# Attention with two gated MLPs on one core: three score products instead of four, one scaling copy less per query head, and another order of the first loads

## The chip, the cores and the metric

The kernel runs on one core of a Trainium2 chip. The metric is the device time of one execution in microseconds, lower is better. Before the change three executions took 1159.36, 1161.23 and 1161.65 us (median 1161.23).

## What is computed

Four batches of eight heads with 576 positions and head size 64, then two MLPs over the 2304 tokens. All arrays are float32.

```python
def _attn_ref(q, k, v, tau):
    scale = 1.0 / np.sqrt(q.shape[-1])
    scores = scale * np.matmul(q, k.transpose(0, 1, 3, 2))
    thresh = np.max(scores, axis=-1, keepdims=True) - tau
    scores = np.where(scores >= thresh, scores, -1000000000.0)
    scores = scores - np.max(scores, axis=-1, keepdims=True)
    attn = np.exp(scores)
    attn = attn / (np.sum(attn, axis=-1, keepdims=True) + 1e-09)
    return np.matmul(attn, v)
# x = attention as [tokens, 512]; x = gate1(x @ w_in) @ w_out; x = gate2(x @ w2_in) @ w2_out
# gate1(h) = h * clip(h + 3, 0, 6) / 6; gate2(h) = h * sigmoid(1.702 * h); hidden size 2048
```

## The kernel before, in words

**Precision.** TensorE multiplies fp32r values, which hold less than float32. Every operand is therefore split: a high part is the value rounded to fp32r, a low part is what the rounding left. A product of two split operands is then made of several matmuls that add up in one PSUM bank: high by high, high by low, low by high.

**The score product.** A head is only 64 rows deep and the array 128, so the kernel puts the query twice into the 128 partitions, and the key too (`load_q`, `load_k`: two transfers each, one per half of the partitions). For a query head three operations make `q_sp`: ScalarE's `high_q` (L700) writes the rounded, scaled query, negated in rows 0 to 63 (scale column `q_hi_scale`); ScalarE's `scale_q` (L704) multiplies `q_raw` by `q_in_scale`, which is 0 in rows 0 to 63 and the scale in rows 64 to 127; GpSimd's `low_q` (L851) subtracts the one from the other. What is left is the high part in rows 0 to 63 and the low part in rows 64 to 127. For a key head ScalarE's `high_k` (L709) and GpSimd's `low_k` (L856) write `k_hi` and `k_lo`, each with the same content in both halves. One matmul of `q_sp` with `k_hi` and one with `k_lo`, both over 128 rows, give all four products (L451).

**Slots.** The 32 heads are taken in 16 pairs. A pair has nine slots of 128 queries: four of its first head, a middle slot (MID) in which the last 64 queries of the first head and the first 64 of the second share the tile, and four of the second head. A slot has four score matmuls of 288 columns (two halves of the keys, `k_hi` and `k_lo`), the MID slot eight: 320 with `k_hi` and 320 with `k_lo` in all 144 slots. Each engine has its program written out by hand, slot by slot, and semaphores tie them. In iteration g of that loop, TensorE makes the scores of slot g+2, turns the masked exponentials of slot g-2 (five 128x128 transposes into `tr`, L466), multiplies a finished group of turned columns by the values (L480) and, from slot 46 on, adds one piece of the first MLP (twelve matmuls of 288 columns, L489 or L498). VectorE takes the row maximum (L590), the mask with its sum (L598) and the low part of the turned columns (L616). ScalarE takes the exponential (L720), the high part of the turned columns (L725) and the high parts of heads, values, weights and x. GpSimd makes the thresholds (L867) and the other low parts.

**Queues around the change.** There are two score buffers, so the scores of slot g+2 wait for the mask of slot g. SyncE issues all transfers; `load_q(h)` and `load_k(h)` wait until head h-2 has been split. Before slot 0 SyncE issues tau, q of head 0, k of head 0, waits for the constants, then v, k and q of head 1. ScalarE starts with L700, L704 and L709 of head 0, takes two exponentials, and then head 1. GpSimd makes the low parts of q and k of head 0, two thresholds, then head 1. TensorE begins when both low parts of head 0 are done. In the loop, pair i+1 is prepared in pair i: `high_k` in slots 2 and 6, `high_q` in 3 and 7, `scale_q` in 4 and 8. At the end of a pair VectorE inverts the nine sums (L605, L607), and TensorE turns them with a transpose whose weight load has nine columns (L459).

**After the attention** (from about 500 us) the rest of the two MLPs runs as plain tiles; no instruction of the change lies there.

The two constants that the split of a query needs:

```python
for half, scale in ((0, -float(HD) ** -0.5), (HD, float(HD) ** -0.5)):
    rows = slice(half, half + HD)
    dve.tensor_scalar(q_hi_scale[rows, :], tau_raw[rows, :], 0.0, scale, ALU.is_ge, ALU.mult)
    dve.tensor_scalar(q_in_scale[rows, :], tau_raw[rows, :], 0.0, max(scale, 0.0), ALU.is_ge, ALU.mult)
```

Of the kernel before, what the change touches and what calls it, by code (L numbers as in the profile page):

```python
# [7 lines left out]
ALU = mybir.AluOpType  # L8
# [3 lines left out]
P = 128  # L12
# [8 lines left out]
def attention_moe_kernel(nc, qT, kT, v, tau, w1_in, w1_out, w2_in, w2_out, out):  # L21
# [81 lines left out]
    with ExitStack() as ctx:  # L103
# [7 lines left out]
        three = sb("three", [P, 1])  # L111
        stage = sb("stage", [P, 2, UNIT])
# [18 lines left out]
        q_hi_scale = sb("q_hi_scale", [P, 1], where=att)  # L131
        q_in_scale = sb("q_in_scale", [P, 1], where=att)
# [38 lines left out]
        q_scaled = sem("q_scaled")  # L171
# [100 lines left out]
        def _(sp):  # L272
            def load_q(h):
                wait(sp, q_lo_done, h - 1)
                for half in range(2):
                    sp.dma_start(q_raw[half * HD:half * HD + HD, h % 2, :], qT[h]).then_inc(q_loaded[h % 2], 16)

            def load_k(h):
                wait(sp, k_lo_done, h - 1)
                for half in range(2):  # L280
                    sp.dma_start(k_raw[half * HD:half * HD + HD, h % 2, :], kT[h]).then_inc(k_loaded[h % 2], 16)
# [153 lines left out]
        def _(pe):  # L435
            def scores(g):
                i, s = divmod(g, SLOTS)
                wait(pe, mask_done, g - 1)
                if s in (0, MID):
                    pe.wait_ge(q_lo_done, 2 * i + 1 + s // MID)  # L440
                    pe.wait_ge(k_lo_done, 2 * i + 1 + s // MID)
# [127 lines left out]
        def _(dve):  # L569
            dve.memset(q_sp[:, S:S + TAIL].bitcast(F32), 0.0).then_inc(consts_done, 1)  # L570
            dve.memset(prob[:, :, S:WIDE], 0.0).then_inc(consts_done, 1)
            dve.memset(v_raw[:, FULL, :], 0.0).then_inc(consts_done, 1)
            dve.memset(three[:, :], 3.0).then_inc(consts_done, 1)
# [4 lines left out]
            for half, scale in ((0, -float(HD) ** -0.5), (HD, float(HD) ** -0.5)):  # L578
                rows = slice(half, half + HD)
                dve.tensor_scalar(q_hi_scale[rows, :], tau_raw[rows, :], 0.0, scale, ALU.is_ge, ALU.mult  # L580
                                  ).then_inc(tau_done, 1)
                dve.tensor_scalar(q_in_scale[rows, :], tau_raw[rows, :], 0.0, max(scale, 0.0), ALU.is_ge, ALU.mult
                                  ).then_inc(tau_done, 1)
            dve.wait_ge(tau_done, 1)
            dve.tensor_tensor(tau_abs[:, :], tau_raw[:, :], tau_neg[:, :], ALU.max).then_inc(tau_done, 1)

# [100 lines left out]
        def _(act):  # L687
# [9 lines left out]
            def high_q(h):  # L697
                act.wait_ge(q_loaded[h % 2], 32 * (h // 2 + 1))
                heads_free(h)
                act.activation(q_place(h), q_raw[:, h % 2, :], ACT.Copy, scale=q_hi_scale[:, :]).then_inc(q_hi_done, 1)  # L700

            def scale_q(h):
                act.wait_ge(q_hi_done, h + 1)
# [266 lines left out]
```

## Time and profile before

| | |
|---|---|
| median of three executions | 1161.23 us (1159.36 to 1161.65) |
| the profiled execution | 1159.2 us, its span 1157.4 us |
| TensorE matmul busy | 1093.3 us, 94% |
| VectorE, ScalarE, GpSimd busy | 560.6, 550.1, 490.9 us |
| chain that ended last | TensorE 82%, VectorE 6%, issue 4%, ScalarE 4%, GpSimd 2%, DMA 1% |

The span runs from the first to the last instruction of the profiled execution. Busy time is the union of an engine's instructions; it does not say whether the engine was the one that others waited for. The chain goes back from the last instruction, at each step to what released it, and so tells which engine set the time in each stretch. In a row of the timeline the first number is the start in the span, the second the duration, and brackets hold the idle time of the engine before it and what ended it. TensorE's matmuls are pipelined: a duration is longer than the distance to the next start, and the distance is what a matmul costs in a dense stretch.

### The profile page before, as it was taken

To read this page: it belongs to the slowest core of one execution; us is meant where nothing else is said; L and a number is where in the kernel's file an instruction comes from. 1 tells how busy PE (TensorE), PEld (TensorE's weight loads), DVE (VectorE), ACT (ScalarE), POOL (GpSimd) and SP (SyncE) were. 2 spreads that over 40 slices of the span, in tenths; PEclk is the share of its full clock that TensorE was granted. 3 is DMA by queue.
4 is the path that set the end of the run, shared out by engine and by line. 5 is a ranking of instruction groups with operands and counts; after the bars stand their busy time and mean duration, and the time that the engine had idled before them with its cause. 6 is when DMAs were issued, how large, how long until landed. Compare 5 with 4: busy or idle time off the path is not lost.

```text
span 1157.4 us, 17664 instructions
## 1 busy us (share of the span) xinstructions
PE 1093.3 (94%) x6720; PEld 1027.0 (89%) x6720; DVE 560.6 (48%) x1038; ACT 550.1 (48%) x1034; POOL 490.9 (42%) x582
## 2 busy tenths in 40 slices
PE   4888799999999999878999999999999999999998
PEld 3767599999999989878999999999999999999997
DVE  3889788778877887224322222232222223222221
ACT  4788686867676776235423333333233223332221
POOL 3466655455645563268333332243333222222222
PEclk9999899999999999989999999999999999999999
DMA  3445563256335522454333211222221002222210
GB/s 109 120 129 151 137 143 103 77 134 169 89 93 134 144 74 77 114 139 141 112 119 118 88 60 54 83 91 91 92 91 55 28 28 82 83 82 82 82 55 27
DMA packets 90627, 112.36 MB, mean 97 GB/s; under 512 B 25120, under 2 KB 69296, under 8 KB 90544
## 3 DMA queue, kind: packets, MB, share of 16 engines
q1 hardware_dynamic: 90544, 111.25, 33.3%
q8 instruction: 53, 0.87, 0.3%
q14 instruction: 30, 0.25, 0.1%
HBM read 78.12 MB, written 33.10 MB: 96 GB/s over the span
## 4 chain that ended last, share of the span: by engine, by line
PE 82%; DVE 6%; issue 4%; ACT 4%; POOL 2%; DMA 1%; SPq 0%; ACTq 0%; POOLq 0%; DVEq 0%
PE mm L489 19%; PE score L500 17%; PE tr L489 13%; PE score L498 10%; PE score L451 7%; PE tr L466 6%; PE mm L480 5%; PE mm L498 5%; DVE prob L598 2%; DVE neg_max L590 2%; DVE pt_lo L616 1%; POOL w_lo L884 1%; ACT gate L749 1%; POOL g_lo L894 1%; DMA inv_b<-inv_scratch 1%
## 5 line engine op out<-in xcount | busy, mean ns | idle before, releaser
L894 POOL TENSOR_TENSOR g_lo<-act_f,g_hi 128x384 fp32r<-128x384 f32 (+1 forms) x208 | 197.7, 955 | 421.5 <-ACT g_hi L757 421.5
L489 PE MATMUL mm<-x_hi,w_hi 128*128 128x384 f32 (+1 forms) x512 | 163.7, 320 | 7.9 <-DVE x_lo L622 7.9
L489 PE MATMUL mm<-x_hi,w_lo 128*128 128x384 f32 (+1 forms) x512 | 162.8, 318 | 0.0
L489 PE MATMUL mm<-x_lo,w_hi 128*128 128x384 f32 (+1 forms) x512 | 162.7, 318 | 0.0
L725 ACT ACTIVATE pt_hi<-tr 128x640 fp32r<-128x640 f32 x144 | 101.7, 706 | 96.5 <-PE tr L466 95.7
L752 ACT ACTIVATE gate<-mm 128x384 f32<-128x384 f32 x48 | 23.6, 492 | 220.5 <-PE mm L489 220.5
L451 PE MATMUL score<-k_hi,q_sp 128*128 128x288 f32 x320 | 98.8, 324 | 29.9 <-DVE prob L598 18.6
L616 DVE TENSOR_TENSOR pt_lo<-tr,pt_hi 128x640 fp32r<-128x640 f32 x144 | 118.3, 821 | 16.2 <-ACT pt_hi L725 14.9
L590 DVE TENSOR_REDUCE neg_max<-score 128x1 f32<-128x576 f32 x144 | 108.2, 751 | 31.1 <-PE score L451 28.3
L867 POOL TENSOR_SCALAR thresh<-neg_max,tau_abs 128x1 f32<-128x1 f32 x144 | 42.0, 292 | 186.3 <-DVE neg_max L590 185.4
L466 PE MATMUL tr<-ident,prob 128*128 128x128 f32 x720 | 106.9, 281 | 14.7 <-issue 12.3
L598 DVE SCALAR_TENSOR_TENSOR prob<-score,thresh,prob 128x576 f32<-128x576 f32 x144 | 116.3, 808 | 0.0
L720 ACT ACTIVATE prob<-score,neg_max 128x576 f32<-128x576 f32 x144 | 106.4, 739 | 13.7 <-DVE neg_max L590 12.9
L500 PE MATMUL score<-w_lo,g_hi 128*128 128x512 f32 x288 | 112.3, 390 | 0.0
L500 PE MATMUL score<-w_hi,g_lo 128*128 128x512 f32 x288 | 112.2, 390 | 0.0
L500 PE MATMUL score<-w_hi,g_hi 128*128 128x512 f32 x288 | 112.0, 389 | 0.0
L757 ACT ACTIVATE g_hi<-act_f 128x384 fp32r<-128x384 f32 (+1 forms) x208 | 102.6, 493 | 8.7 <-DVE act_f L630 6.2
L466 PEld LDWEIGHTS tr<-ident,prob 128*128 128x128 f32 x720 | 84.1, 144 | 24.8 <-issue 23.5
L489 PEld LDWEIGHTS mm<-x_hi,w_hi 128*128 128x128 f32 x512 | 96.7, 189 | 10.0 <-issue 8.1
L489 PE MATMUL tr<-x_hi,w_hi 128*128 128x384 f32 (+1 forms) x320 | 105.6, 330 | 0.0
L489 PE MATMUL tr<-x_lo,w_hi 128*128 128x384 f32 (+1 forms) x320 | 105.6, 330 | 0.0
L489 PE MATMUL tr<-x_hi,w_lo 128*128 128x384 f32 (+1 forms) x320 | 105.6, 330 | 0.0
(73 smaller groups left out, 2439.8 us busy)
## 6 DMA issues: line engine op xcount, KB each, us to landing
x_raw<-x_t_scratch SPq DMA_DIRECT2D x18, 768.0 KB, 6.2
q_raw<-in_qT SPq DMA_DIRECT2D x64, 144.0 KB, 2.9
k_raw<-in_kT SPq DMA_DIRECT2D x64, 144.0 KB, 2.8
stage<-in_w_in SPq DMA_DIRECT2D x16, 512.0 KB, 6.8
stage<-in_w_out SPq DMA_DIRECT2D x16, 512.0 KB, 7.1
o_parts_scratch<-o_t SPq DMA_DIRECT2D x32, 160.0 KB, 1.8
x_raw<-o_parts_scratch SPq DMA_DIRECT2D x16, 288.0 KB, 5.3
part<-o_parts_scratch SPq DMA_DIRECT2D x16, 288.0 KB, 6.2
```

Of the source, the lines that this page charges most:

```text
L451: m = pe.matmul(score[:, g % 2, half, 0:HALF], q_sp[:, col:col + P], k_part[:, side, half * HALF:half * HALF + HALF], start=e == 0, stop=e ...
L466: m = pe.transpose(turned_p[:, c * P:c * P + P], prob[:, x % PROBS, c * P:c * P + P], ident[:, :])
L489: m = pe.matmul(bank[:, 0:width], w[:, col:col + P], x[:, k, 0:width], start=(k == 0 and e == 0), stop=(k == KC - 1 and e == 2))
L498: r = pe.matmul(bank[:, 0:width], w[:, col + m * P:col + m * P + P], g[:, c, 0:width], **ends)
L500: r = pe.matmul(bank[:, :], g[:, c, m * P:m * P + P], w[:, col:col + DM], **ends)
L590: dve.tensor_reduce(neg_max[:, r:r + 1], score[:, g % 2, :, 0:HALF], AX.XY, ALU.max, negate=True).then_inc(max_done, 1)
L598: dve.scalar_tensor_tensor(out=p, in0=score[:, g % 2, :, 0:HALF], scalar=thresh[:, r:r + 1], in1=p, op0=ALU.is_ge, op1=ALU.mult, accum_out ...
L616: dve.tensor_tensor(pt_place(pt_lo, x), turned_place(x), pt_place(pt_hi, x), ALU.subtract).then_inc(pt_lo_done, 1)
L720: act.activation(prob[:, g % PROBS, 0:S].rearrange("p (a n) -> p a n", a=2), score[:, g % 2, :, 0:HALF], ACT.Exp, bias=neg_max[:, r:r + 1] ...
L725: act.activation(pt_place(pt_hi, x), turned_place(x), ACT.Copy).then_inc(pt_hi_done, 1)
L757: act.activation(g_hi[:, c, 0:width], act_f[:, c % 2, 0:width], ACT.Copy).then_inc(g_hi_done, 1)
L894: pool.tensor_tensor(g_lo[:, c, 0:width], act_f[:, c % 2, 0:width], g_hi[:, c, 0:width], ALU.subtract).then_inc(g_lo_done, 1)
```

## The change

- The scale 1/8 goes into the high parts of both sides. `q_scale` is 1 in rows 0 to 63 and the scale in rows 64 to 127, `k_scale` the other way round. `high_q` writes the rounded value with that column, and `low_q` subtracts only rows 0 to 63. `q_sp` then holds the low part, not scaled, above, and the scaled high part below; `k_hi` holds the scaled high part above and the plain one below. `scale_q` is gone.
- `k_lo` is valid only in rows 64 to 127, and the matmul with it takes these 64 rows alone. Low by low is no longer computed: three products instead of four. The number of matmuls and their columns stay as they were.
- `high_k` has a scale column now. The first key head is split by VectorE.
- q and k of a head come by one transfer each, whose source gives each row twice. The first loads stand in the order q0, tau, k0, k1, q1.
- ScalarE makes one exponential of a constant column before anything else. On ScalarE and GpSimd, head 1 stands ahead of the first exponentials and thresholds.

```diff
-                for half in range(2):
-                    sp.dma_start(q_raw[half * HD:half * HD + HD, h % 2, :], qT[h]).then_inc(q_loaded[h % 2], 16)
+                sp.dma_start(q_raw[:, h % 2, :], both_halves(qT[h])).then_inc(q_loaded[h % 2], 16)
...
+            load_q(0)
             sp.dma_start(tau_raw[:, :], tau.broadcast_to([P, 1])).then_inc(tau_loaded, 16)
-            load_q(0)
             load_k(0)
+            load_k(1)
+            load_q(1)
             sp.wait_ge(consts_done, 8)
             load_v(0)
-            load_k(1)
-            load_q(1)
...
-                parts = [(side, col, k_part) for side, col in sides for k_part in (k_hi, k_lo)]
+                parts = [(side, col, k_part, rows) for side, col in sides for k_part, rows in ((k_hi, 0), (k_lo, HD))]
                 for half in range(2):
-                    for e, (side, col, k_part) in enumerate(parts):
-                        m = pe.matmul(score[:, g % 2, half, 0:HALF], q_sp[:, col:col + P],
-                                      k_part[:, side, half * HALF:half * HALF + HALF],
+                    for e, (side, col, k_part, rows) in enumerate(parts):
+                        m = pe.matmul(score[:, g % 2, half, 0:HALF], q_sp[rows:P, col:col + P],
+                                      k_part[rows:P, side, half * HALF:half * HALF + HALF],
...
+            dve.wait_ge(k_loaded[0], 16)
+            dve.tensor_scalar(k_hi[:, 0, :], k_raw[:, 0, :], k_scale[:, :], None, ALU.mult).then_inc(first_k_hi_done, 1)
+            dve.wait_ge(first_k_hi_done, 1)
+            dve.tensor_tensor(k_lo[:, 0, :], k_raw[:, 0, :], k_hi[:, 0, :], ALU.subtract).then_inc(first_k_lo_done, 1)
...
-            def scale_q(h):
-                act.wait_ge(q_hi_done, h + 1)
-                act.activation(q_raw[:, h % 2, :], q_raw[:, h % 2, :], ACT.Copy, scale=q_in_scale[:, :]).then_inc(q_scaled, 1)
...
-                act.activation(k_hi[:, h % 2, :], k_raw[:, h % 2, :], ACT.Copy).then_inc(k_hi_done, 1)
+                act.activation(k_hi[:, h % 2, :], k_raw[:, h % 2, :], ACT.Copy, scale=k_scale[:, :]).then_inc(k_hi_done, 1)
...
+            act.activation(warm[:, :], three[:, :], ACT.Exp)
             act.wait_ge(tau_done, 6)
             high_q(0)
-            scale_q(0)
-            high_k(0)
+            high_k(1)
+            high_q(1)
             exponent(0)
             exponent(1)
-            high_k(1)
-            high_q(1)
-            scale_q(1)
...
-                pool.wait_ge(q_scaled, h + 1)
-                pool.tensor_tensor(q_sp[:, first:first + S], q_raw[:, h % 2, :], q_sp[:, first:first + S], ALU.subtract
-                                   ).then_inc(q_lo_done, 1)
+                pool.wait_ge(q_hi_done, h + 1)
+                pool.tensor_tensor(q_sp[0:HD, first:first + S], q_raw[0:HD, h % 2, :], q_sp[0:HD, first:first + S],
+                                   ALU.subtract).then_inc(q_lo_done, 1)
...
             low_q(0)
-            low_k(0)
+            low_k(1)
             threshold(0)
             threshold(1)
-            low_k(1)
             low_q(1)
```

The start of ScalarE's program, with the semaphores that each instruction waits for, before and then with the change:

```order
L700 ACT_TABLE_LOAD [waits q_loaded0,tau_done]
L700 ACTIVATE q_sp<-q_raw,q_hi_scale 128x576 [waits consts_done]
L704 ACTIVATE q_raw<-q_raw,q_in_scale 128x576 [waits q_hi_done]
L709 ACTIVATE k_hi<-k_raw 128x576 [waits k_loaded0]
L720 ACTIVATE prob<-score,neg_max 128x576 [waits max_done] x2
L709 ACTIVATE k_hi<-k_raw 128x576 [waits k_loaded1]
L700 ACTIVATE q_sp<-q_raw,q_hi_scale 128x576 [waits q_loaded1]
L704 ACTIVATE q_raw<-q_raw,q_in_scale 128x576 [waits q_hi_done]
L720 ACTIVATE prob<-score,neg_max 128x576 [waits max_done] x2
```

```order
L774 ACT_TABLE_LOAD
L774 ACTIVATE warm<-three 128x1 [waits consts_done]
L717 ACTIVATE q_sp<-q_raw,q_scale 128x576 [waits q_loaded0,tau_done]
L722 ACTIVATE k_hi<-k_raw,k_scale 128x576 [waits k_loaded1]
L717 ACTIVATE q_sp<-q_raw,q_scale 128x576 [waits q_loaded1]
L733 ACTIVATE prob<-score,neg_max 128x576 [waits max_done] x4
```

The table load has left the place behind the first query's arrival and waits for nothing; the key of head 0 is gone from ScalarE, and head 1 stands ahead of the first exponentials.

GpSimd behind its constants, before and then with the change (L851 and L859 are `low_q`, L856 and L864 `low_k`, L867 and L875 the threshold):

```order
L851 TENSOR_TENSOR q_sp<-q_raw,q_sp 128x576
L856 TENSOR_TENSOR k_lo<-k_raw,k_hi 128x576
L867 TENSOR_SCALAR thresh<-neg_max,tau_abs 128x1 x2
L856 TENSOR_TENSOR k_lo<-k_raw,k_hi 128x576
L851 TENSOR_TENSOR q_sp<-q_raw,q_sp 128x576
```

```order
L859 TENSOR_TENSOR q_sp<-q_raw,q_sp 64x576
L864 TENSOR_TENSOR k_lo<-k_raw,k_hi 128x576
L875 TENSOR_SCALAR thresh<-neg_max,tau_abs 128x1 x2
L859 TENSOR_TENSOR q_sp<-q_raw,q_sp 64x576
```

The first key split (k of head 0) left for VectorE; the one that stands second now is head 1's, and it stands ahead of the first threshold.

ScalarE in slots 7 and 8 of the first pair, where the second head of the next pair is prepared, before and then with the change:

```order
L700 ACTIVATE q_sp<-q_raw,q_hi_scale 128x576
L725 ACTIVATE pt_hi<-tr 128x5x128
L720 ACTIVATE prob<-score,neg_max 128x576
L704 ACTIVATE q_raw<-q_raw,q_in_scale 128x576
L731 ACTIVATE o_t<-mm 128x320
L725 ACTIVATE pt_hi<-tr 128x5x128
```

```order
L717 ACTIVATE q_sp<-q_raw,q_scale 128x576
L738 ACTIVATE pt_hi<-tr 128x5x128
L733 ACTIVATE prob<-score,neg_max 128x576
L744 ACTIVATE o_t<-mm 128x320
L738 ACTIVATE pt_hi<-tr 128x5x128
```

The scaling copy between the exponential and `o_t` is gone, and nothing else moved.

## Rows read from the trace of the kernel before

**Rows 1.** Windows: per stretch its us, busy per engine (x instructions), PEclk, DMA, GB/s

```profile
10.00:33.00 23.00, 16.57 (x64) 14.17 (x65) 13.26 (x24) 11.34 (x18) 7.86 (x13) 1.00 0.33 93
60.00:90.00 30.00, 26.01 (x168) 21.28 (x168) 27.35 (x53) 25.58 (x43) 19.58 (x26) 1.00 0.49 136
145.00:205.00 60.00, 59.05 (x451) 57.36 (x450) 49.04 (x97) 44.30 (x82) 32.84 (x47) 1.00 0.47 124
```

**Rows 2.** Timeline of the start: start us, us, engine line op, names, shapes [idle before <-releaser]

```profile
0.74 0.40 SPq L357 DMA_DIRECT2D tau_raw<-in_tau  x1
1.20 1.18 SPq L276 DMA_DIRECT2D q_raw<-in_qT  x2
...
4.05 0.16 DVE L585 TENSOR_TENSOR tau_abs<-tau_raw,tau_neg 128x1 f32<-128x1 f32 x1
...
4.80 1.28 ACT L700 ACT_TABLE_LOAD   x1 [4.80 <-DMA q_raw<-in_qT]
...
6.09 0.77 ACT L700 ACTIVATE q_sp<-q_raw,q_hi_scale 128x576 fp32r<-128x576 f32 x1
...
7.85 1.40 POOL L851 TENSOR_TENSOR q_sp<-q_raw,q_sp 128x576 fp32r<-128x576 f32 x1 [5.95 <-ACT q_raw L704]
9.21 1.40 POOL L856 TENSOR_TENSOR k_lo<-k_raw,k_hi 128x576 fp32r<-128x576 f32 x1
...
10.75 0.58 PE L451 MATMUL score<-k_hi,q_sp 128*128 128x288 f32 x1 [10.75 <-POOL k_lo L856]
...
11.37 0.44 PE L451 MATMUL score<-k_hi,q_sp 128*128 128x288 f32 x1
...
11.61 0.44 PE L451 MATMUL score<-k_lo,q_sp 128*128 128x288 f32 x1
```

**Rows 3.** Transfers into q_raw up to 40 us, and the window from 3 to 4 us

```profile
DMA to landing us min/median/max: 2.7/2.9/3.0
...
3.00:4.00 1.00, 0.00 (x0) 0.00 (x0) 0.46 (x5) 0.00 (x0) 0.00 (x0) 1.00 0.78 251
```

**Rows 4.** Timeline, the same VectorE operation alone and beside a GpSimd operation

```profile
199.49 0.17 DVE L605 TENSOR_SCALAR total_e<-total 128x9 f32<-128x9 f32 x1
...
229.66 0.65 DVE L605 TENSOR_SCALAR total_e<-total 128x9 f32<-128x9 f32 x1
...
229.47 0.81 POOL L894 TENSOR_TENSOR g_lo<-act_f,g_hi 128x288 fp32r<-128x288 f32 x1 [0.79 <-ACT g_hi L757]
```

**Rows 5.** Groups by line and shape: busy us, mean ns of one | idle before

```profile
L622 DVE TENSOR_TENSOR x_lo<-x_raw,x_hi 128x384 fp32r<-128x384 f32 x72 | 51.2, 769 | 18.0 <-ACT x_hi L744 18.0
...
L704 ACT ACTIVATE q_raw<-q_raw,q_in_scale 128x576 f32<-128x576 f32 x32 | 24.7, 772 | 0.1
L700 ACT ACTIVATE q_sp<-q_raw,q_hi_scale 128x576 fp32r<-128x576 f32 x32 | 24.6, 770 | 0.0
L709 ACT ACTIVATE k_hi<-k_raw 128x576 fp32r<-128x576 f32 x32 | 21.9, 684 | 0.0
```

**Rows 6.** Waits from 145 to 470 us: us in total, times, longest

```profile
PE score L451 <- DVE prob L598: 8.0, 11, 1.2
```

**Rows 7.** Timeline of ScalarE, VectorE and TensorE around one of these waits

```profile
426.72 0.78 ACT L704 ACTIVATE q_raw<-q_raw,q_in_scale 128x576 f32<-128x576 f32 x1
...
427.86 0.49 DVE L622 TENSOR_TENSOR x_lo<-x_raw,x_hi 128x288 fp32r<-128x288 f32 x1 [0.41 <-ACT x_hi L744]
...
430.17 0.40 PE L451 MATMUL score<-k_hi,q_sp 128*128 128x288 f32 x1 [0.86 <-DVE prob L598]
```

**Rows 8.** Timeline of TensorE, dense, around the transpose with nine weight columns

```profile
443.67 0.29 PE L451 MATMUL score<-k_hi,q_sp 128*128 128x288 f32 x1
443.80 0.29 PE L451 MATMUL score<-k_lo,q_sp 128*128 128x288 f32 x1
443.93 0.27 PE L459 MATMUL tr<-ident,inv_total 128*9 128x128 f32 x1
444.04 0.71 PE L466 MATMUL tr<-ident,prob 128*128 128x128 f32 x5
```

More of the change, by code:

```diff
@@ L130, in attention_moe_kernel @@
         tau_abs = sb("tau_abs", [P, 1], where=att)
-        q_hi_scale = sb("q_hi_scale", [P, 1], where=att)
-        q_in_scale = sb("q_in_scale", [P, 1], where=att)
+        q_scale = sb("q_scale", [P, 1], where=att)
+        k_scale = sb("k_scale", [P, 1], where=att)
         q_raw = sb("q_raw", [P, 2, S], where=att)
@@ L272, in _, with both_halves @@
         def _(sp):
+            def both_halves(rows):
+                return bass.AP(tensor=rows.tensor, offset=rows.offset, ap=[[0, 2]] + [list(a) for a in rows.ap])
             def load_q(h):
                 wait(sp, q_lo_done, h - 1)
-                for half in range(2):
-                    sp.dma_start(q_raw[half * HD:half * HD + HD, h % 2, :], qT[h]).then_inc(q_loaded[h % 2], 16)
+                sp.dma_start(q_raw[:, h % 2, :], both_halves(qT[h])).then_inc(q_loaded[h % 2], 16)
             def load_k(h):
-                wait(sp, k_lo_done, h - 1)
-                for half in range(2):
-                    sp.dma_start(k_raw[half * HD:half * HD + HD, h % 2, :], kT[h]).then_inc(k_loaded[h % 2], 16)
+                if h == 2:
+                    sp.wait_ge(first_k_lo_done, 1)
+                else:
+                    wait(sp, k_lo_done, h - 2)
+                sp.dma_start(k_raw[:, h % 2, :], both_halves(kT[h])).then_inc(k_loaded[h % 2], 16)
             def load_v(h):
@@ L440, in scores @@
                     pe.wait_ge(q_lo_done, 2 * i + 1 + s // MID)
-                    pe.wait_ge(k_lo_done, 2 * i + 1 + s // MID)
+                    if g == 0:
+                        pe.wait_ge(first_k_lo_done, 1)
+                    else:
+                        pe.wait_ge(k_lo_done, 2 * i + s // MID)
                 if s < MID:
@@ L572, in _ @@
             dve.memset(v_raw[:, FULL, :], 0.0).then_inc(consts_done, 1)
-            dve.memset(three[:, :], 3.0).then_inc(consts_done, 1)
             dve.wait_ge(tau_loaded, 16)
-            dve.tensor_scalar(tau_neg[:, :], tau_raw[:, :], -1.0, None, ALU.mult).then_inc(tau_done, 1)
[L578 to L584, printed above, removed]
+            for tile, half in ((q_scale, HD), (k_scale, 0)):
+                rows, others = slice(half, half + HD), slice(HD - half, P - half)
+                dve.tensor_scalar(tile[rows, :], tau_raw[rows, :], 0.0, float(HD) ** -0.5, ALU.is_ge, ALU.mult
+                                  ).then_inc(tau_done, 1)
+                dve.memset(tile[others, :], 1.0).then_inc(tau_done, 1)
+            dve.tensor_scalar(tau_neg[:, :], tau_raw[:, :], -1.0, None, ALU.mult).then_inc(tau_done, 1)
+            dve.wait_ge(tau_done, 5)
             dve.tensor_tensor(tau_abs[:, :], tau_raw[:, :], tau_neg[:, :], ALU.max).then_inc(tau_done, 1)
+            dve.wait_ge(k_loaded[0], 16)
+            dve.tensor_scalar(k_hi[:, 0, :], k_raw[:, 0, :], k_scale[:, :], None, ALU.mult).then_inc(first_k_hi_done, 1)
+            dve.wait_ge(first_k_hi_done, 1)
+            dve.tensor_tensor(k_lo[:, 0, :], k_raw[:, 0, :], k_hi[:, 0, :], ALU.subtract).then_inc(first_k_lo_done, 1)
             def row_max(g):
@@ L791, in _ @@
                         high_q(2 * i + 2)
-                    if s == 4 and i + 1 < PAIRS:
-                        scale_q(2 * i + 2)
                     if s == 5:
@@ L799, in _ @@
                         high_q(2 * i + 3)
-                    if s == 8 and i + 1 < PAIRS:
-                        scale_q(2 * i + 3)
                     if s in (0, 5) and 0 < i <= UNITS:
```

13 lines of the change are left out of this document (8 added, 5 removed).

## The prediction
> **What bounds the kernel now.** I read the windows first, for how full each engine is in each stretch, then the timeline of the start, then the waits and the timeline of the stretch in which attention and MLP are mixed. Three stretches matter. Before the first matmul everything is a serial chain, and TensorE starts at 10.75 us [rows 2]. From there to about 145 us (46 slots, no MLP work) VectorE is the fullest engine, 27.35 of 30 us, with TensorE at 26.01 and ScalarE at 25.58 [rows 1]. From 145 to about 470 us (98 slots) TensorE is busy 59.05 of 60 us, ScalarE only 44.30 [rows 1]. Behind that no instruction of the change runs. So ScalarE, from which the change takes most, bounds no long stretch; what counts is the start, the few waits of TensorE, and whether the score matmuls still cost what they did.
>
> **Part 1: the start.** Before: tau goes first (issued 0.74), q0 second (1.20); the table load sits behind q0's landing at 4.80 and takes 1.28, then L700 (0.77), `scale_q` and `high_k` on ScalarE, then 1.40 + 1.40 us of GpSimd, then TensorE at 10.75 [rows 2]. After, each step at its duration in these rows:
> - q0 is issued at 0.74 in one transfer. A transfer of 144 KB took 2.9 us from its issue; one of 288 KB needs at the 251 GB/s of the loading phase some 0.6 us more [rows 3]. q0 lands at about 4.2, tau right behind it, 4.3. k0 is limited by the same rate: 1.2 us later, 5.4. k1 follows at 6.6, q1 at 7.8.
> - The table load waits for nothing and is over long before 4.3: 1.28 us go off the path. The exponential of one column hides there too.
> - Six small VectorE operations took until 4.21 from tau's landing, some 0.7 us (the last ran from 4.05 for 0.16) [rows 2]. ScalarE's L700 then runs from 5.0 to 5.8, and GpSimd's `low_q` from 5.9 for 1.40 us. It has half the rows, but the same columns, so I take the same duration: 7.3. `scale_q`, 0.77, is gone from the path.
> - VectorE splits k0 beside that: two operations of 576 columns. The nearest row is 769 ns for a subtraction of 384 columns, in a mean that includes waiting [rows 5]; I take 0.7 us each, from 5.45 to 6.9.
> - The second of them and `low_q` want SBUF at the same time. The addition to nine sums takes 0.17 us alone and 0.65 us when a GpSimd subtraction started 0.19 us before it, and it ends as that one ends [rows 4]. So one of the two waits for the other: the later one ends at about 8.0 in place of 7.3. The Trainium skill (SBUF — State Buffer, "SBUF: two separate sides") says that a VectorE operation with two SBUF inputs and a GpSimd operation take the shared port pair as an exclusive lock; by it alone the start would be at about 8.1, without it at 7.4. The row agrees.
> - First matmul at 7.9, against 10.75: **-2.9 us**. Ends: 7.4 if the two do not meet and the transfers land as early as small ones did (-3.4), 8.8 if both meet in full and k0 lands 0.7 us later (-2.0).
>
> Behind the first matmul two things are queued that were not. ScalarE has k1 and q1 (0.77 each, k1's landing 6.6) ahead of the first exponential: done at 8.6, while the first row maximum cannot be there before 9.9. GpSimd has `low_k(1)` (1.40) ahead of the first threshold: from 8.0 to 9.4, again before 9.9. Cost nothing; if k1 lands over 0.5 us late the difference comes back as delay of slot 0.
>
> **Part 2: slots without MLP work.** 11 of the 32 `scale_q` lie here. VectorE at 91% is the bound and loses no instruction. I read a whole pair on the timeline: ScalarE had ended `scale_q` before the transposes that it waits for next were done, in slots 4 and 8 alike. 0 us.
>
> **Part 3: slots with MLP work.** TensorE waited 8.0 us here in 11 places, all ahead of scores whose mask was late [rows 6]. A wait gets shorter only if ScalarE was late because of `scale_q`. One case is in rows 7: `scale_q` at 426.72, then x's high part, VectorE idle 0.41 us for it, and the scores 0.86 us late: 0.41 us come back. Two more places on the timeline have such a VectorE idle, 0.15 and 0.22 us; in the others VectorE had no idle time before the late mask, since it was inverting the sums. **-0.8 us**. Bounds: 0, if the next wait ends as late; -5.4, if each wait with a `scale_q` in its slot gave back up to the 0.67 us between two starts on ScalarE.
>
> **Part 4: what is added or only moved.** `high_k` gets a scale column: 770 ns with one (L700), 684 without (L709) [rows 5], so 31 times 0.09 us on ScalarE, which has over 15 of 60 us free in the mixed stretch: 0. In all ScalarE loses 24.7 us and gains 2.7. The first key is split by VectorE, in idle time. One transfer in place of two moves the same bytes and saves SyncE about 0.6 us each (1.18 for two [rows 2]); no transfer of q or k is waited for behind the start: 0.
>
> **Part 5: the matmul with 64 rows.** 320 of the 640 score matmuls use rows 64 to 127 only. Their columns stay 288, and in a dense stretch the distance between two starts is 0.13 us for 288 columns [rows 8], so fewer rows gain nothing. They alternate with matmuls of 128 rows, which makes 640 changes of the array's shape. No row of this kernel shows a change of rows. The nearest is a change of columns: the transpose with nine weight columns starts 0.13 us behind the score matmul, as all do, and the next starts 0.11 us behind it [rows 8]. Nothing is lost there, and I take 0. The other end is below, as a rival. The Trainium skill (TensorEngine Tiling (Array Packing), "Key Properties") says that a change of the tiling mode drains TensorE, and it lists both kinds as modes. For columns the rows speak against it; for rows no row here shows it. By that rule the sum would be rival A's.
>
> **Sum.** -2.9 - 0.8 = -3.7 us: the profiled execution, 1159.2 us, becomes 1155.5. That execution is 2.0 us below the median of 1161.23; the four known times lie at 1159.2 and 1159.36 and at 1161.23 and 1161.65, two and two. I put the forecast for a median between: 1156.5 us (1155.5 by the one base, 1157.5 by the other). About 0.2%, 2.3 us, is what a measurement can tell from no change. Own range of this case: 1153 to 1159.
>
> **Rival A, slower: the change of rows stops TensorE.** Before each change the array would first have to give out what is in it. Price per change, from rows: a matmul takes 0.29 us to its results where the next starts after 0.13, so a full drain costs 0.16; a matmul behind an idle time took 0.40 in place of 0.29, so a restart costs 0.11 [rows 7, 8]. In the mixed slots TensorE is the bound; they hold 98 x 4 + 11 x 4 = 436 changes: 48 us at 0.11. All 640 at 0.16 make 102 us. The time would be 1156.5 + 48 = 1204 up to 1258, and for a shorter stop of p us about 436 to 640 p more. It decides from p = 3.7 / 640 = 0.006 us on. For it: two shapes alternate in one accumulation, which this kernel never did. Against: rows 8. Chance of a p over 0.006: 0.23, of which 0.09 below 0.04 us.
>
> **Rival B, slower: the clock.** At 11 us 288 columns took 0.24 us, the level of 1.2 GHz; later they take 0.13, the level of 2.4 GHz [rows 2, 8]; the mean matmul is busy for 0.26 us from 10 to 33 us (16.57 for 64) and for 0.15 from 60 to 90 (26.01 for 168) [rows 1]. On the timeline the change comes after 31 us, when the value products had begun. Half as many rows at work might put it off. Some 37 slots without MLP work lie behind it; each has 4.4 score matmuls that would be 0.11 slower, 0.5 us, and the row maximum waits for them: up to 18 us, about 1174. Against: TensorE is busy for the same share of the time. Chance 0.05.
>
> **Rival C, nothing to be seen.** The start is earlier but the gain is eaten: the clock rises at the same absolute time, so some 3 us more run at the low level (0.5 us), k0 and `low_q` meet in full (0.9 us less), and the mixed slots give nothing: -3.7 + 0.5 + 0.9 + 0.8 = -1.5, or 1159.7. Chance 0.14.
>
> **How the numbers follow.** Forecast 0.58, rivals A 0.23, B 0.05, C 0.14. Faster by over 0.2% (below 1158.9): 0.95 of the forecast's 0.58 and a sixth of C, 0.58. Slower (over 1163.5): A without its smallest stops, and B, 0.26. The rest, 0.16, within 0.2%. The range starts at 1153 and reaches to 1176, a stop of 0.03 to 0.04 us per change or B's price; what is left out is 0.03 below and about 0.15 above, the large stops of A.
>
> **What would show it.** Right: the first score matmul starts between 7.4 and 8.8; starts of score matmuls in a dense stretch remain 0.13 apart, with `k_hi` and with `k_lo`; ScalarE's busy time falls by some 22 us and TensorE's stays; the waits before scores in the mixed stretch drop by about 0.8 from 8.0 us. Wrong: distances over 0.14 at every change of rows (A), distances of 0.24 beyond 35 us (B), or a start before 8 with the 46th slot no earlier than before (C).

## The result, and the profile after

The changed kernel takes 1281.73 us (median of four, 1280.09 to 1284.99), the kernel before 1161.44 beside it: ratio 1.1039, 95% interval 1.1008 to 1.1069. It is 120 us slower, and outside the range given.

The page of the changed kernel, busy time by engine and the chain that ended last. In all views PE stands for TensorE's matmuls, PEld for its weight loads, DVE for VectorE, ACT for ScalarE, POOL for GpSimd and SPq for what SyncE issues; a window gives busy time in the order PE, PEld, DVE, ACT, POOL, then the granted clock (PEclk), the DMA share and GB/s.

```profile
span 1279.8 us, 17569 instructions
PE 1208.4 (94%) x6720; PEld 1059.7 (83%) x6720; DVE 570.2 (45%) x1040; ACT 529.3 (41%) x1002; POOL 488.0 (38%) x581
...
PE 85%; DMA 4%; DVE 4%; issue 3%; POOL 2%; ACT 1%; SPq 1%; ACTq 0%; DVEq 0%; POOLq 0%
```

ScalarE lost 21 us of busy time, as forecast. TensorE has as many matmuls as before and is busy 115 us longer. TensorE has 85% of the chain (82% before), and DMA rose from 1% to 4%. So two things are to be found: why TensorE takes longer for the same matmuls, and which transfers are waited for.

**TensorE.** The timeline of the changed kernel in a dense stretch answers to [rows 8]:

```profile
300.12 0.29 PE L500 MATMUL mm<-x_hi,w_lo 128*128 128x288 f32 x1
300.12 0.19 PEld L462 LDWEIGHTS score<-k_hi,q_sp 128*128 128x128 f32 x1
300.25 0.29 PE L462 MATMUL score<-k_hi,q_sp 128*128 128x288 f32 x1
...
300.47 0.18 PEld L462 LDWEIGHTS score<-k_lo,q_sp 64*128 64x128 f32 x1 [0.16 <-issue]
300.47 0.40 PE L462 MATMUL score<-k_lo,q_sp 64*128 64x288 f32 x1
300.80 0.19 PEld L462 LDWEIGHTS score<-k_hi,q_sp 128*128 128x128 f32 x1
300.80 0.40 PE L462 MATMUL score<-k_hi,q_sp 128*128 128x288 f32 x1
301.12 0.18 PEld L462 LDWEIGHTS score<-k_lo,q_sp 64*128 64x128 f32 x1
301.12 0.40 PE L462 MATMUL score<-k_lo,q_sp 64*128 64x288 f32 x1
301.45 0.14 PEld L477 LDWEIGHTS tr<-ident,prob 128*128 128x128 f32 x1
301.45 0.33 PE L477 MATMUL tr<-ident,prob 128*128 128x128 f32 x1
```

The starts are 0.22, 0.33, 0.32 and 0.33 us apart where they were 0.13 apart. Look at the weight loads. The load of the first score matmul (300.12) stands beside the matmul ahead of it, 0.13 us early. Every load behind a change of rows starts together with its own matmul and is no longer hidden. That the nine-column transpose costs nothing still holds: its successor starts 0.11 us behind it, at full rows on both sides.

```profile
304.40 0.28 PE L470 MATMUL tr<-ident,inv_total 128*9 128x128 f32 x1
304.51 0.60 PE L477 MATMUL tr<-ident,prob 128*128 128x128 f32 x4
```

**The transfers.** SyncE and the first matmul on the timeline of the changed kernel, which answers to [rows 2]:

```profile
0.73 0.71 SPq L281 DMA_DIRECT2D q_raw<-in_qT  x1
1.51 0.41 SPq L365 DMA_DIRECT2D tau_raw<-in_tau  x1
...
1.96 4.30 SPq L288 DMA_DIRECT2D k_raw<-in_kT  x2
...
6.30 5.43 SPq L281 DMA_DIRECT2D q_raw<-in_qT  x1
10.51 0.77 ACT L717 ACTIVATE q_sp<-q_raw,q_scale 128x576 fp32r<-128x576 f32 x1 [8.28 <-DVE tau_abs L596]
...
11.78 5.57 SPq L293 DMA_DIRECT2D v_raw<-in_v  x1
15.18 0.52 DVE L600 TENSOR_SCALAR k_hi<-k_raw,k_scale 128x576 fp32r<-128x576 f32 x1 [4.71 <-DMA k_raw<-in_kT]
...
16.64 0.58 PE L462 MATMUL score<-k_hi,q_sp 128*128 128x288 f32 x1 [16.64 <-DVE k_lo L602]
```

The first matmul starts at 16.64 us, not at 7.9. k0 landed at about 15.2 and q1 at 26.85, 20.55 us after its issue; the third slot (slot 2 of pair 0) began at 29.19 (14.60 before), since `high_q(1)` stands ahead of the first exponentials on ScalarE. The windows of the changed kernel show how little the 16 DMA engines did meanwhile, against the 251 GB/s of [rows 3]:

```profile
3.00:4.00 1.00, 0.00 (x0) 0.00 (x0) 0.00 (x0) 0.00 (x0) 0.00 (x0) 1.00 0.16 51
10.00:33.00 23.00, 6.56 (x13) 3.44 (x13) 5.48 (x12) 4.32 (x6) 5.01 (x6) 1.00 0.16 56
```

A share of 0.16 is two and a half of the 16 engines. What is queued behind such a transfer comes late too. Stores of attention's output, with their size and the median us from issue to landing (before: 1.8 us):

```profile
o_parts_scratch<-o_t SPq DMA_DIRECT2D x32, 160.0 KB, 8.0
```

**Where the 122 us lie.** From the start of the first score matmul of each pair on the timelines (pair 15 ends here with the start of its last slot); differences to the kernel before, in us, of one profiled execution each. Pairs 0 to 4 have no MLP work, 6 to 15 are mixed with it, and in pair 5 the mixing begins. The columns add up to the difference of the profiled spans. Executions of one kernel lie several us apart, so differences of 1 or 2 us in a span say nothing; a3's profiled execution, 1162.87 us, is among the slowest of its twelve. The kernels below the first row are those of the experiments.

| kernel | first matmul | pairs 0-4 | pair 5 | pairs 6-14 | pair 15 | behind | span |
|---|---|---|---|---|---|---|---|
| before, us | 10.8 | 116.3 | 36.4 | 269.6 | 27.0 | 697.3 | 1157.4 |
| changed | +5.9 | +40.6 | +10.0 | +59.1 | +5.9 | +1.0 | +122.4 |
| a1_rows128 | +5.9 | +35.7 | +8.8 | +37.0 | 0 | +1.4 | +88.8 |
| a2_two_loads | -2.0 | +40.4 | +0.4 | +54.1 | +5.9 | +1.5 | +100.3 |
| a3_both | -2.0 | +0.8 | +0.5 | +2.9 | 0 | +1.5 | +3.7 |
| b1_rows64 | 0 | +35.1 | +1.9 | +53.7 | +5.9 | -0.1 | +96.5 |
| b2_one_load | +7.5 | +37.4 | +7.6 | +41.2 | 0 | -0.1 | +93.6 |
| b3_spread | -0.1 | +0.6 | +0.3 | +0.2 | 0 | +0.8 | +1.7 |
| a4_grouped | -2.1 | +6.0 | +0.9 | +18.8 | +2.2 | +0.3 | +26.1 |
| c1_tau_first | -2.3 | -1.9 | +0.3 | +3.1 | 0 | +0.3 | -0.5 |

### The profile page after: what moved, and what is told of

Same layout as the page of the kernel before. It is cut to its first block, busy times and chain, and to the rows that moved or that the text cites. A ratio compares the mean times of both kernels' runs of the same rounds, so it can differ in the third digit from the quotient of the medians.

```text
span 1279.8 us, 17569 instructions
## 1 busy us (share of the span) xinstructions
PE 1208.4 (94%) x6720; PEld 1059.7 (83%) x6720; DVE 570.2 (45%) x1040; ACT 529.3 (41%) x1002; POOL 488.0 (38%) x581
## 4 chain that ended last, share of the span: by engine, by line
PE 85%; DMA 4%; DVE 4%; issue 3%; POOL 2%; ACT 1%; SPq 1%; ACTq 0%; DVEq 0%; POOLq 0%
PE mm L500 18%; PE score L511 15%; PE score L462 15%; PE tr L500 12%; PE score L509 10%; PE tr L477 5%; PE mm L509 5%; PE mm L491 5%; DVE prob L615 3%; DMA q_raw<-in_qT 2%; DMA o_parts_scratch<-o_t 1%; POOL w_lo L892 1%; POOL g_lo L902 1%; DMA inv_b<-inv_scratch 1%; DMA v_raw<-in_v 1%
## 5 line engine op out<-in xcount | busy, mean ns | idle before, releaser
L462 PE MATMUL score<-k_hi,q_sp 128*128 128x288 f32 x320 | 123.8, 387 | 42.4 <-DVE prob L615 23.0
L875 POOL TENSOR_SCALAR thresh<-neg_max,tau_abs 128x1 f32<-128x1 f32 x144 | 42.0, 292 | 281.3 <-DVE neg_max L607 280.9
L462 PE MATMUL score<-k_lo,q_sp 64*128 64x288 f32 x320 | 132.0, 413 | 0.0
L462 PEld LDWEIGHTS score<-k_hi,q_sp 128*128 128x128 f32 x320 | 63.0, 197 | 82.7 <-DVE prob L615 38.8
L477 PE MATMUL tr<-ident,prob 128*128 128x128 f32 x720 | 113.8, 291 | 9.3 <-issue 9.2
L615 DVE SCALAR_TENSOR_TENSOR prob<-score,thresh,prob 128x576 f32<-128x576 f32 x144 | 116.3, 807 | 6.5 <-ACT prob L733 6.5
```

The lines of the kernel that those rows point to most:

```text
L462: m = pe.matmul(score[:, g % 2, half, 0:HALF], q_sp[rows:P, col:col + P], k_part[rows:P, side, half * HALF:half * HALF + HALF], start=e == ...
L477: m = pe.transpose(turned_p[:, c * P:c * P + P], prob[:, x % PROBS, c * P:c * P + P], ident[:, :])
L615: dve.scalar_tensor_tensor(out=p, in0=score[:, g % 2, :, 0:HALF], scalar=thresh[:, r:r + 1], in1=p, op0=ALU.is_ge, op1=ALU.mult, accum_out ...
```

## Two causes, taken away one at a time

Theory 1: the change of rows costs some 0.2 us each. Theory 2: the single transfers, whose source repeats 64 rows, are served slowly.

**a1_rows128**: the changed kernel without the change of rows. The added rows multiply the unused half of `k_lo` with the low part of q, so the values differ; no work is left out.

```
-for k_part, rows in ((k_hi, 0), (k_lo, HD))
+for k_part, rows in ((k_hi, 0), (k_lo, 0))
```

> The changed kernel, but the matmul with k_lo takes all 128 rows again, so that all 640 score matmuls have one shape. (Rows 0 to 63 of k_lo hold no low part, so the values change; no work is left out.) Theory 1, each change between 64 and 128 rows costs TensorE about 0.19 us: score matmuls start 0.13 us apart in dense stretches, and some 105 us go (83 from 436 changes in mixed slots, the rest from the slots without MLP work): 1172 to 1182 us, still slower than before by the slow first loads. Rival, the slow transfers of q and k make the loss: above 1250 us.

**a2_two_loads**: the changed kernel with two transfers of 64 rows each for q and k.

```
-sp.dma_start(q_raw[:, h % 2, :], both_halves(qT[h]))
+for half in range(2):
+    sp.dma_start(q_raw[half * HD:half * HD + HD, h % 2, :], qT[h])
```

> The changed kernel, but q and k of a head come by two transfers of 64 rows each again; order of loads and all else as changed. Theory 2, a transfer whose source starts with a step of zero over two is served by few DMA engines: the first score matmul starts at 8 to 9 us in place of 16.6, slot 2 at 12 to 13 in place of 29.2, SyncE's issues take 0.6 us again, and the wait for v behind the first x loads shrinks; in all 18 to 27 us less than the changed kernel, 1255 to 1264 us. The distance between score matmuls stays 0.32. If the rival (transfers make the whole loss) holds: below 1175.

**a3_both**: both alterations together.

> Both: 128 rows for k_lo and two transfers of 64 rows. What is left of the change is the scale in the high parts, one ScalarE operation for a query, the first key on VectorE, the order of the first loads and the early table load. Both theories, and parts 1 to 3 of the prediction: 3.7 us under the kernel before, about 1157 to 1158 us, ratio 0.996 to 0.998, first score matmul at 7.4 to 8.8 us. If these parts are worth nothing: ratio 1.000.

Measured: a1 1248.04 us, a2 1259.51 (one run each), a3 1160.61, beside 1159.87 for the kernel before. a3's ratio is 0.9999 (0.9988 to 1.001): not the 3.7 us that parts 1 to 3 promised, but the other case, in which they are worth nothing. So the two causes together are the whole loss. Each alone costs 88 or 100 us, and both together 122, not 188. a2's time came as expected, though its slot 2 began at 14.71 us and not at 12 to 13. a1 fits neither expectation (it lies 2 us under the rival's): I had taken the loss of the transfers for a matter of the start. The waits of a1 from 12 to 470 us show a loss all along:

```profile
ACT v_hl L727 <- DMA v_raw<-in_v: 54.4, 12, 13.5
PEld tr L477 <- issue: 43.4, 32, 14.2
```

and its transfers, KB each and us to landing:

```profile
v_raw<-in_v SPq DMA_DIRECT2D x32, 16.0 KB, 9.2
```

ScalarE stands for v up to 13.5 us, and the evictions of the transposes stand behind it. In the changed kernel TensorE is slower, and the same late v is waited for less: 17.5 us in all, in 4 places. The causes overlap.

Part of what late transfers cost comes by way of TensorE's clock. Up to the last score matmul the granted clock was at half for 6.8 us in the kernel before, for 82 in a1, 96 in b2 (below) and 34 in the changed kernel; in a1 the first such stretches come behind idle times of TensorE of 2 to 3 us (from 51.3, 71.3 and 81.7 us), and the longest falls into one of 14.0 us (from 169.5). The same window in a1 and in the kernel before:

```profile
105.00:127.00 22.00, 18.07 (x97) 16.36 (x98) 16.08 (x31) 14.23 (x24) 11.64 (x16) 0.77 0.33 112
```

```profile
105.00:127.00 22.00, 18.92 (x123) 15.30 (x122) 20.56 (x39) 17.11 (x28) 13.38 (x17) 1.00 0.67 163
```

TensorE is almost as busy, with 97 matmuls in place of 123. It was busy for 54 us of a1's time at the low level, against 5 before; work at half the clock takes twice as long, so I estimate that up to 25 of the 88 us are of this kind (29 in b2, 10 in the changed kernel). No run takes the clock out by itself.

Put in the other way, each cause alone into the kernel before:

**b1_rows64**: the second score product over rows 0 to 63 only, which leaves out the product of the two low parts.

```
-m = pe.matmul(score[...], q_sp[:, col:col + P], k_part[:, side, ...]
+m = pe.matmul(score[...], q_sp[0:rows, col:col + P], k_part[0:rows, side, ...]
```

> The kernel before, with one edit: the matmul with k_lo takes rows 0 to 63 only (the high part of q; the product low by low is left out). The 64 rows lie at the other end of the array than in the change. Theory 1: score matmuls start 0.32 us apart in dense stretches, slot distance without MLP work about 2.95 in place of 2.54 us, 100 to 110 us slower than before, 1261 to 1272 us. If only the place in rows 64 to 127 costs: no change, 1161.

**b2_one_load**: the single transfers alone, in the kernel before.

> The kernel before with one alteration: q and k of each head come by one transfer whose source repeats 64 rows (its first dimension has two entries), in place of two. Theory (such a transfer is served by about two of the 16 DMA engines, at some 50 GB/s, holds SyncE for 3 to 6 us at its issue, and makes what is queued behind it late): 1230 to 1262, with q and k landing over 6 us after their issue and output stores landing at a median of over 6 us; first matmul later than 14 us. Rival (it costs only together with the changed order at the start, where four of them stand in a row): under 1180.

Measured: b1 1255.77 us, b2 1252.77 (one run each, the kernel before at 1159.87 and 1159.66). b1 is a little under its range; the timeline has the same distances as the changed kernel, with the other half of the array:

```profile
301.12 0.29 PE L451 MATMUL score<-k_hi,q_sp 128*128 128x288 f32 x1
301.35 0.39 PE L451 MATMUL score<-k_lo,q_sp 64*128 64x288 f32 x1
301.67 0.40 PE L451 MATMUL score<-k_hi,q_sp 128*128 128x288 f32 x1
302.00 0.39 PE L451 MATMUL score<-k_lo,q_sp 64*128 64x288 f32 x1
302.32 0.77 PE L466 MATMUL tr<-ident,prob 128*128 128x128 f32 x5
```

b2 lies within its range, so the rival (only together with the new order at the start) falls. Its start moved by 7.5 us although tau landed 2.6 us after its issue: q0 landed at 10.1 and k0 at 16.0, on the timeline:

```profile
10.13 1.28 ACT L701 ACT_TABLE_LOAD   x1 [10.13 <-DMA q_raw<-in_qT]
...
15.99 0.68 ACT L710 ACTIVATE k_hi<-k_raw 128x576 fp32r<-128x576 f32 x1 [2.98 <-DMA k_raw<-in_kT]
```

## What makes a matmul slow: the rows, or their change

**a4_grouped**: a2 with the score matmuls in another order, k_hi for both halves, then k_lo for both: as many 64-row matmuls, fewer changes.

```
-for half in range(2):
-    for e, (side, col, k_part, rows) in enumerate(parts):
+parts.sort(key=lambda x: x[3])
+for e, (side, col, k_part, rows) in enumerate(parts):
+    for half in range(2):
```

> The changed kernel with two 64-row transfers for q and k, and its score matmuls in another order: first the two halves with k_hi (128 rows), then the two with k_lo (rows 64 to 127). As many 64-row matmuls as before, but two changes of rows per slot in place of four. The same kernel with the halves alternating measured 1259.5, 98 us over the kernel before. Theory 1 (each change of rows costs about 0.2 us, since the weights of the next matmul are then not loaded ahead): half of it goes, 1204 to 1216; in a dense slot the starts stand 0.32, 0.13, 0.32, 0.13 us apart. Rival (each 64-row matmul is slow by itself, by twice that amount, and the changes are free): 1252 to 1264.

Measured: 1185.21 us (1184.77 to 1186.99), ratio 1.0226 (1.0208 to 1.0243). The rival (64-row matmuls are slow by themselves) falls; theory 1 stands, but its figure was at least 19 us too high. Three reasons. Slot 4 of a pair has eight score matmuls, and its changes fall from eight to two, so a pair has 18 changes in place of 40, not half. In pairs 0 to 4 the changes left, 18 of them at about 0.17 us, 3 us a pair, find room in TensorE's idle time, also some 3 us of a pair's 22.8: VectorE bounds them again, at 26.75 of 30 us, as before [rows 1]. And two changes in a row of like matmuls cost a dense slot 0.33 us and not 0.40, as the timeline below shows. Windows of a2 and of a4:

```profile
60.00:90.00 30.00, 27.29 (x137) 18.78 (x135) 22.84 (x44) 20.36 (x34) 16.22 (x21) 1.00 0.38 108
```

```profile
60.00:90.00 30.00, 27.25 (x160) 20.53 (x161) 26.75 (x51) 23.48 (x39) 19.68 (x25) 1.00 0.47 134
```

TensorE is equally busy in both, with 137 matmuls in a2 and 160 in a4: in a2 VectorE waits for it. a4's timeline, dense, where x2 joins two matmuls of the same shape:

```profile
300.37 0.42 PE L465 MATMUL score<-k_hi,q_sp 128*128 128x288 f32 x2
...
300.72 0.29 PEld L465 LDWEIGHTS score<-k_lo,q_sp 64*128 64x128 f32 x2 [0.16 <-issue]
300.72 0.53 PE L465 MATMUL score<-k_lo,q_sp 64*128 64x288 f32 x2
...
301.18 0.42 PEld L480 LDWEIGHTS tr<-ident,prob 128*128 128x128 f32 x4 [0.17 <-issue]
```

Two k_hi take 0.35 us to the next start, two k_lo 0.46. Over the mixed stretch the median distances are 0.13 from k_hi to k_hi, 0.22 to the first k_lo, 0.24 to the second, 0.22 to the transpose. I read this as two prices per change: 0.09 us in which the next matmul can't start, and 0.10 us of a weight load that stands in the open. The load of the second k_lo, where nothing changes, is hidden again: it starts at 300.83, its matmul at 300.96. A dense slot then has 0.33 us more than before (3.59 in place of 3.26), and the changed kernel 0.73 (3.99). Split in this way the two prices are an inference; that the sum belongs to the change is shown. a2 beside a4 settles it: from a k_lo to the transpose behind it takes 0.33 us in a2, where that k_lo itself follows a change, and 0.22 in a4, where it follows another k_lo; and in a2 the second k_hi, of 128 rows, is as slow to its successor (0.33) as any k_lo.

## What makes the transfer slow

**b3_spread**: the kernel before with single transfers of the same bytes and descriptors, whose source runs over the rows first and repeats second. Rows come to lie in pairs, so the values differ; no work is left out.

```
-ap=[[0, 2]] + [list(a) for a in rows.ap]
+ap=[list(rows.ap[0]), [0, 2], list(rows.ap[1])]
```

> The kernel before with q and k by one transfer each, of the same bytes and descriptors as in the other single transfer, but its source runs over the 64 rows first and repeats each row second (so partitions 2r and 2r+1 get row r, and the values computed are others; no work is left out). Theory (the first dimension of the pattern sets over how many DMA engines a transfer is spread: 2 entries give two engines, 64 give all): landings of 3 to 4 us as before, 1158 to 1163, ratio 0.997 to 1.002. Rival (a source that reads the same rows twice in one transfer is slow, or 128 descriptors in one transfer are): 1230 or more.

Measured: 1161.19 us, ratio 1.0014 (1.0004 to 1.0025). The rivals fall: 128 descriptors in one transfer and rows that are read twice cost at most 0.25% together, where b2 lost 8%. DMA up to 30 us, in b2 and in b3 (KB each, us to landing, and the queue's packets, MB and share of the 16 engines):

```profile
DMA packets 1324, 1.45 MB, mean 48 GB/s; under 512 B 761, under 2 KB 761, under 8 KB 1324
q1 hardware_dynamic: 1323, 1.45, 14.1%
```

```profile
DMA packets 2700, 3.28 MB, mean 109 GB/s; under 512 B 1504, under 2 KB 1504, under 8 KB 2700
q1 hardware_dynamic: 2700, 3.28, 40.0%
k_raw<-in_kT SPq DMA_DIRECT2D x5, 288.0 KB, 3.2
q_raw<-in_qT SPq DMA_DIRECT2D x4, 288.0 KB, 3.4
```

Each transfer of q or k took 3.2 to 3.4 us here, and its bytes came at up to 335 GB/s in a part of that window; with two entries in the first dimension the queue took 14% of the 16 engines, about two. The Trainium skill (DMA: Bandwidth & Descriptors, "Rules for kernel authors") says this too: an outermost dimension of c entries, a leading repetition among them, confines the whole transfer to at most c engines. The runs agree: from 4 to 6 us the DMA share was 0.13 in b2 and 0.98 in b3. SyncE is held as well: in the changed kernel its issues at the start took 3.7 to 5.6 us each once some transfers were queued, 0.6 us in b3.

## What is left of the gain, and where it goes

With both causes undone the start is 2.0 us earlier and nothing remains. I tried for a version that keeps it.

**c1_tau_first**: a3 with tau issued ahead of q0.

> The changed kernel with both costs undone (128 rows for k_lo, two transfers each for q and k), and tau issued first, ahead of q0. In the one with q0 first, tau was issued at 2.00 us, landed at about 4.8 and set the start of ScalarE (5.80) and the first matmul (8.79). Theory (the rest of the start is real but does not last): first matmul at 7.9 to 8.3, and yet 1158 to 1163, ratio 0.997 to 1.001, because the slots without MLP give the lead back. Rival (what is gained at the start stays): 2.4 to 2.8 us under the kernel before, ratio 0.9976 to 0.9979.

**d1_v_between**: the kernel before, with v's loads moved into the loads of x.

```
 for a in range(2):
+    if a == 1:
+        load_v(2 * i + 1)
     side = slice(a * HD, a * HD + HD)
```

> The kernel before with one move in SyncE's order: in each of the three places where six loads of x stand ahead of the two loads of v for the next head (288 KB each against 144 KB together), v goes between the third and the fourth of them. In the trace of before v landed 7.5 us after its issue there, ScalarE waited for it 4.8, 0.7 and 0.9 us, and at 133 us TensorE stood idle 5.56 us behind it. Theory (v's landing ends those waits, and the queue in front of it sets the landing): 1155 to 1158, 2 to 4.5 us below the kernel before; TensorE's idle time at 133 us falls to 1 to 4 us. Rival (x is wanted as early, and lands later by what v gains): within 1 us of the kernel before.

**d2_tau_v**: the same in c1.

> The same move of v's loads in the changed kernel with both costs undone and tau issued first. That one led the kernel before by 4.1 us at the fourth pair, and lost 2.2 us of it in the first slot of pair 9 (5.62 us in place of 3.47), where ScalarE waited 3.1 us for v and held up the transposes' evictions. Theory (late v loads take the lead away): slot 81 back to 3.4 to 4.0 us, the waits at 130 us shorter too, 1152 to 1156. Rival (the lead is lost wherever the next transfer or eviction is late): 1158 to 1161, level with the kernel before.

Measured: c1 1160.43 us, ratio 1.0011 (1.0 to 1.0022); d1 1162.24, ratio 1.001 (0.9999 to 1.0022); d2 1160.92, ratio 0.9999 (0.9988 to 1.001). c1 is level with the kernel before, as expected, but not for the reason given: the slots without MLP work kept its lead. The first matmul came at 8.47 us in c1, a little later than expected, since VectorE's first operation on k0 took 1.60 us beside GpSimd (0.52 in a3):

```profile
5.82 1.39 POOL L861 TENSOR_TENSOR q_sp<-q_raw,q_sp 64x576 fp32r<-64x576 f32 x1 [3.91 <-ACT q_sp L719]
5.93 1.60 DVE L602 TENSOR_SCALAR k_hi<-k_raw,k_scale 128x576 fp32r<-128x576 f32 x1 [1.47 <-DMA k_raw<-in_kT]
```

c1's lead grew from 2.3 to 4.1 us by the fourth pair, was 3.8 at pair 9, and 1.55 at pair 10. The growth was luck: in this execution TensorE reached the level of 0.13 us for 288 columns at 22.3 us, in d2, whose program is the same up to there, at 31.4, and d2's lead stayed at 2.3 over the first pair. A wait of c1 from 248.7 to 281.8 us:

```profile
ACT v_hl L729 <- DMA v_raw<-in_v: 3.1, 1, 3.1
```

In the kernel before the same wait was 0.7 us. A store of 160 KB had landed 3.5 us after its issue in place of 1.8, SyncE's loads of x wait for it, and v stands behind them. So 2.2 us of the lead are lost to a late transfer, and d2, with v earlier, loses only 0.4 there. But d1 and d2 show that v alone isn't the cause to remove: with v earlier, x is waited for. The waits of d1 from 118 to 260 us:

```profile
PE score L454 <- DVE prob L601: 7.2, 8, 3.8
DVE x_lo L625 <- ACT x_hi L747: 6.8, 7, 3.0
...
POOL x_raw L879 <- DMA inv_b<-inv_scratch: 4.9, 2, 4.6
```

TensorE's idle time of 5.56 us at 133 us became two, 1.62 us before 128.5 and 3.77 before 133.8, so hardly less in all, and the slot behind got longer (4.72 us in place of 3.51); the granted clock was at half for 10.2 us there, for 6.8 before. In d2 slot 81 took 3.87 us, within the expectation, and by then the lead was already down to 0.1. The rivals of d1 and d2 hold, d1 at 1.02 us from the kernel before. Part of d2's lead went between 60 and 90 us, where the granted clock was 0.92 (1.00 in c1); what puts a stretch of the lower level there I can't say. A lead of 2.3 us is thus as large as what such stretches add or take from one execution to the next.

## Why the prediction was wrong

- **Part 5, 0 us: the step that failed first.** I took a change of rows at nothing because a change of columns costs nothing. The changed kernel shows 0.20 us for a change inside the group and 0.09 for the first behind a dense stretch: 0.73 us in a dense slot, 100 us in a2. The rule of the Trainium skill (TensorEngine Tiling (Array Packing), "Key Properties"), that a change of the tiling mode drains TensorE, is borne out for rows by these timelines (0.09 us to the next start, and the weight load in the open). For columns the transpose shows no loss, but no run shows whether a weight load of nine columns is such a change at all. I let one kind of change stand for the other.
- **Rival A** had the mechanism and gave 1204 to 1258; a2, with this cost alone, measured 1259.5. Its two prices (0.16 for a drain, 0.11 for a restart) were put as alternatives, and its lower end counted only the slots where TensorE was already the bound. Both prices were too low, since the weight load comes into the open, and pairs 0 to 4, at 26.01 of 30 us, had no room for eight changes' worth of them in slot 4 and four in each other slot: +40 us.
- **Part 4, 0 us: the second step that failed.** "The same bytes" was true, and no measure of the time. The transfer got about two of 16 engines; Part 1's landing times (4.2, 5.4, 6.6, 7.8) became up to 26.85. Alone, this costs 88 to 93 us. The 288 KB of k0 need some 6 us at the 49 to 52 GB/s that the traces now show (an estimate), in place of the 1.2 in the sum. The rule of the Trainium skill on a first dimension of two (DMA: Bandwidth & Descriptors, "Rules for kernel authors") stood against the change and was not weighed. No rival had it; the sentence that no transfer of q or k is waited for behind the start left out what is queued behind them.
- **Part 1, -2.9 us**: -2.0 in a3, -2.3 in c1, within the bound that was given (8.8), once the transfers are undone; the changed kernel itself started at 16.64. a3 was short of the forecast by tau, which landed at 4.83 and not at 4.3, and by the six small VectorE operations behind it, which took 0.9 us and not 0.7. The meeting of VectorE and GpSimd the prediction priced about right: in a3 GpSimd's `low_q` took 1.94 us beside VectorE, 1.39 alone. The prediction quoted the rule of the Trainium skill on the shared port pair (SBUF — State Buffer, "SBUF: two separate sides") only for VectorE operations with two SBUF inputs; it names those in a two-port mode as well. The operation of [rows 4] is itself one of a single input, and c1's `k_hi` has one tensor input and a column of scales, took 0.52 us alone for 576 columns where the subtraction took 0.76, and 1.60 beside GpSimd. The trace agrees with the wider rule.
- **Part 2, 0 us**: right, as far as c1 tells; its pairs 1 to 4 take what they did, within 0.2 us in all.
- **Part 3, -0.8 us**: not there. In a3, from 145 to 470 us, TensorE waited 8.9 us for masks in 11 places [rows 6]. Its lower bound, 0, came true: ScalarE lost 18 us of busy time in a3, and TensorE waited no less. That another wait ended as late each time is likely, but I did not follow all eleven.
- **Rival B** had a small part, though not for the reason that it gave; this rests on one execution of each kernel. The level of 2.4 GHz (five transposes in 0.71 to 0.77 us in place of 1.33) was there at 34 us in the kernel before and 32 in a3, but only at 44 in b1, 57 in the changed kernel and 59 in a2. In a4, with as many 64-row matmuls, it was there at 32, so the half of the rows alone doesn't put it off; what in the alternation does, stays open. In a2 pair 1 lost 10.2 us where pairs 2 and 3 lost 5.1 and 6.3: an estimate of 4 to 5 us for the late rise. The later stretches at half the granted clock come on top, above all behind late transfers, as said for a1.
- **Rival C**, a gain that is eaten, describes a3, c1 and d2, whose start gain does not reach the end; eaten by late transfers and stretches at the lower granted clock, which it had not named. Its own term, a clock that rises at the same absolute time, did not come: in a3 and d2 the rise stands in slot 8, as in the kernel before.

## What to carry to other kernels

Evidence from one kind of change (fewer columns) says nothing on another (fewer rows): where a form of instruction alternates with another for the first time, take it as unpriced until a run shows it (0.20 us for each change here, more than either price that I had read from rows), and group the shapes if you must have both. A transfer is judged by how its pattern is dealt out over the engines, not by its bytes: don't lead with a short dimension, and look at the DMA share beside GB/s. Two causes on one path don't add: 88 and 100 us made 122, so undo both before you say what is left. An earlier start is worth only what no late transfer further on takes back. And a wait of the engine that bounds the kernel can cost twice, once as idle time and once as a stretch at the lower clock behind it.

## What the hardware showed that I had not expected

- In these traces a weight load in a dense stretch is hidden behind the matmul ahead only between matmuls of equal rows. Behind a change it starts with its own matmul, 0.14 to 0.19 us in the record. It makes no difference which half of the array the 64 rows lie in (b1 and the changed kernel: 0.32 to 0.33 us).
- In the first slots, at the 1.2 GHz level, the distance with a change of rows was 0.54 us, against 0.24 without [rows 2]. The granted clock of the windows reads 1.00 there, so this level shows only in the distances:

```profile
29.73 0.61 PE L462 MATMUL score<-k_lo,q_sp 64*128 64x288 f32 x1
30.27 0.61 PE L462 MATMUL score<-k_hi,q_sp 128*128 128x288 f32 x1
```

- A source pattern that begins with two entries ran at 49 to 52 GB/s, and delayed other transfers on the queue: tau's 0.5 KB, issued behind q0 in both, landed 8.0 us after its issue in the changed kernel and 2.8 us after it in a3.
